# Pair products of a decaying-state attention: one matmul per head on 64 rows of the array, instead of one per pair of heads on 128 rows

## Chip, cores and metric

The kernel runs on one core of one Trainium2 chip. Its metric is the device time of one execution, in microseconds (us); lower is better.

## What is computed

Three layers follow each other. The first is an attention with a decaying state, over 4 batches, 8 heads, 768 steps and 48 channels per head; the other two are dense layers on the 3072 resulting rows of 384 numbers.

```python
for t in range(S):
    kt, vt, rt, wt = (k[:, :, t], v[:, :, t], r[:, :, t], w[:, :, t])
    cur = np.einsum('bhd,bhe->bhde', u[None] * kt, vt)
    y[:, :, t] = np.einsum('bhd,bhde->bhe', rt, state + cur)
    state = wt[:, :, :, None] * state + np.einsum('bhd,bhe->bhde', kt, vt)
...
h = x @ w_in
g = np.where(pos, h, np.where(neg, 0.0, (h + beta) ** 2 / (4.0 * beta)))
x = g @ w_out
...
h = x @ w_in
g = np.where(h > 0.0, h, alpha * (np.exp(np.minimum(h, 0.0)) - 1.0))
out = g @ w_out
```

## The kernel before, in words

**Stages.** The 768 steps are cut into 6 chunks of 128 (`NC = 6`, `CH = 128`). The attention of chunk 0 runs alone ("stage 0" below). Then `layer1_tile(c, True)` computes the first dense layer of chunk c and, woven into it, the attention of chunk c + 1 (stages 1 to 5, c = 0 to 4). Then come the last tile of the first dense layer without attention, and six tiles of the second dense layer.

**Attention of a chunk.** Each batch has 4 pairs of heads. The 16 pairs of a chunk are split into two groups g of `GP = 8`. The tile `att{g}` holds r, w, k with channels on the partitions, a pair of heads at partitions 0 to 47 and 64 to 111 (`PAD = 64`), and steps along the free dimension. The weight that step s has for step t is a product of decays between them; the kernel reaches it in `NL = 7` levels. At level l, with m = 2**l, steps are grouped in blocks of m, and each product of a k in an even block with an r in the odd block behind it is taken. These are the **pair products** (`pair_products`): TensorE multiplies k (stationary, 128 partitions x 128 steps) with odd steps of r (moving). VectorE (`level`) then multiplies odd r by a decay (L777), copies the products that a mask picks from the two PSUM banks into `a_` (two predicated copies, L780), and multiplies even k by a decay (L784); `next_decays` (L791) follows. The next level of the same group needs the updated r and k.

**The block-diagonal copies.** Before, one matmul takes a pair of heads over all 128 partitions. So that the two heads do not mix, its moving operand is `rbd_`, 128 columns per pair: for the upper 64 partitions the first 64 columns hold the 64 odd steps of r and the rest is zero, for the lower ones the other way round. `odd_blocks` fills it with two copies of 64 partitions x 512 elements per level: ScalarE for level 0 of chunk 0 and for levels 1 to 6 (`next_odd_blocks`), GpSimd (`times_one`, L348) for level 0 of later chunks. `wait_rbd` makes TensorE and VectorE wait for them.

**What orders the work.** Each engine's order is written out by hand. `PLAN` gives the slots f (0 to 15) of a dense tile in which levels stand: group 0 in slots 0, 2, 3, 4, 5, 6, 7 ("early", behind `up(c, f)`), group 1 in slots 5 to 11 ("late", behind `down(c, f - 2)`). Rows of the attention itself (`turn_k`, `attend`, `state_step`) stand in slots 9, 10, 13, 14. In slots 5, 6 and 7 both groups have a level. In later chunks both groups share the banks `g_bank`, so `bank_user` also waits for the other group's predicated copies, one half (one bank) at a time. A dense slot is 9 matmuls `up` (three of the moving 512 columns for each of 3 parts of x) and 9 matmuls `down`.

**DMA.** SyncE issues loads and stores (`load_group`, `reload`, `reload_natural`); the change does not touch them.

Of the kernel before, what the change touches and what calls it, by code (L numbers as in the profile page):

```python
# [34 lines left out]
B, H, S, D = 4, 8, 768, 48  # L35
DM, FF = 384, 2048
P = 128
# [10 lines left out]
NL = 7  # L48
# [17 lines left out]
def build(nc, rT, wT, kT, vN, rN, kN, uN, masks_d, ident_d, w1_in, w1_out, w2_in, w2_out, x2_d, out_d):  # L66
    with ExitStack() as ctx:
# [16 lines left out]
        widths = [NR, NR, NR, NR, NV, NA]  # L84
        att = [sb(f"att{g}", [P, sum(widths)]) for g in range(2)]
        r_, w_, k_, rbd_, v_, a_ = ([a[:, sum(widths[:i]):sum(widths[:i + 1])] for a in att]
# [53 lines left out]
        rbd_zeroed = sem("rbd_zeroed")  # L140
        zeroed = sem("zeroed")
        r0_ready = [sem(f"r0_ready{g}") for g in range(2)]
# [13 lines left out]
        rbd_ready = [sem(f"rbd_ready{g}") for g in range(2)]  # L156
# [67 lines left out]
        def odd_blocks(copy, k, g, l):  # L224


            m = 2 ** l
            for a in range(2):
                ps = slice(a * PAD, (a + 1) * PAD)
                if m < HALF:  # L230
                    out = rbd_[g][ps, :].rearrange("p (n a j m) -> p n a j m", a=2, n=GP, m=m)[:, :, a]
                    in_ = r_[g][ps, :].rearrange("p (n j two m) -> p n j two m", n=GP, two=2, m=m)[:, :, :, 1]
                else:
                    out = rbd_[g][ps, :].rearrange("p (n a m) -> p n a m", a=2, m=m)[:, :, a]
                    in_ = r_[g][ps, :].rearrange("p (n two m) -> p n two m", two=2, m=m)[:, :, 1]
                last = copy(out, in_, ps)
            last.then_inc(rbd_ready[g] if l else r0_ready[g], 1)

        def wait_rbd(engine, k, g, l):

            if l == 0:
                engine.wait_ge(r0_ready[g], k + 1)
            else:
                engine.wait_ge(rbd_ready[g], k * (NL - 1) + l)
# [90 lines left out]
        def _(pool):  # L335
# [9 lines left out]
            def times_one(out, in_, ps):  # L345

                ones = consts[ps, 2:3].rearrange("p (x y z) -> p x y z", x=1, y=1)
                return nc.gpsimd.tensor_tensor(out, in_, ones.broadcast_to(list(in_.shape)), ALU.mult)  # L348

# [20 lines left out]
            for g in range(2):  # L370

                nc.gpsimd.memset(rbd_[g], 0.0).then_inc(rbd_zeroed, 1)
            for g in range(2):
                nc.gpsimd.memset(a_[g], 0.0)
# [12 lines left out]
            with pool.Fori(1, NC) as k:  # L387
                for g in range(2):

                    if g == 0:  # L390
                        pool.wait_ge(w1_lo_ready, len(W1_PIECES))
                        pool.wait_ge(vd_ready[1], k)
                    pool.wait_ge(rk_in[g], k * 32 + 32)
                    pool.wait_ge(g_filled[g], k * NFILL)
                    odd_blocks(times_one, k, g, 0)
                pool.wait_ge(r0_ready[1], k + 1)
                for g in range(2):
                    diagonal_product(k, g)
# [6 lines left out]
        def _(pe):  # L405
# [3 lines left out]
            def pair_products(k, g, l):  # L409

                wait_rbd(pe, k, g, l)
                if l == 0:
                    pe.wait_ge(rk_in[g], k * 32 + 32)
                else:
                    pe.wait_ge(k_updated[g], k * NL + l)
                for half in range(2):
                    bank_user(k, g, l, half)
                    bank_ = product_banks(k, g)[half]
                    for i in range(HP):
                        j = half * HP + i  # L420
                        last = mm(bank_[:, i * P:(i + 1) * P], k_[g][:, j * CH:(j + 1) * CH],
                                  rbd_[g][:, j * P:(j + 1) * P])
                    last.then_inc(g_filled[g], 1)

            def bank_user(k, g, l, half):
# [557 lines left out]
```

## Time and profile before

| | |
|---|---|
| median of 3 runs | 1153.86 us |
| lowest and highest run | 1153.84, 1159.4 us |
| span of the profiled execution | 1154.6 us |
| busy, share of span | TensorE matmul 94%, TensorE weight load 79%, VectorE 57%, ScalarE 50%, GpSimd 12% |
| mean granted TensorE clock | 0.980 of full speed |

The profiled execution has no separate time beside its span; 1154.6 us is the time that the steps below are counted against. PE is TensorE's matmuls, PEld its weight loads, DVE VectorE, ACT ScalarE, POOL GpSimd, SPq SyncE's queue. Matmuls overlap one another in the records, so that the distance from one start to the next tells the pace, and the duration of one does not. A float32 matmul of the program shows as two passes in the trace, each with a weight load and a matmul of its own: the 8 matmuls of a level are 16 records.

### The profile page before, as it was taken

Reading aid. Unit: us, or ns where it says so; the run is one execution under the profiler, and the core shown is the slowest. Engines: PE = TensorE matmul, PEld = TensorE weight load, DVE = VectorE, ACT = ScalarE, POOL = GpSimd, SP = SyncE. Lnnn points to the kernel's source line nnn. Section 1 sums busy time; section 2 is a strip of 40 time slices with the busy share of each in tenths; the row PEclk is TensorE's granted clock in tenths of the full one; section 3 lists DMA queues with packets and bytes.
Section 4 is the critical chain, followed back from the end, with each engine's and each line's share of the span. In section 5 each row is a group of like instructions: output and inputs, shape, how many; then the busy total and the mean of one; then the engine's idle time right before and its main releaser. Section 6 shows DMA issues by size and latency. Waiting matters only on the chain.

```text
span 1154.6 us, 15811 instructions
## 1 busy us (share of the span) xinstructions
PE 1086.5 (94%) x5704; PEld 915.1 (79%) x5704; DVE 655.4 (57%) x962; ACT 573.1 (50%) x959; POOL 139.9 (12%) x96
## 2 busy tenths in 40 slices
PE   4687999899989998999989999999999999999998
PEld 3576898689868887788778888888888888888886
DVE  5996855686568656875687544543333333333332
ACT  3444544564456444544454457664545444454543
POOL 5664100310031003100310000000000000000000
PEclk8798999999999999999989999999999999999999
DMA  7233001400140014001400240010101000010000
GB/s 280 85 112 143 1 1 69 150 0 0 68 150 0 0 68 150 0 0 68 150 0 0 109 164 1 4 51 1 54 0 55 0 19 36 0 54 0 27 0 27
DMA packets 23369, 60.58 MB, mean 52 GB/s; under 512 B 2352, under 2 KB 6832, under 8 KB 22960
## 3 DMA queue, kind: packets, MB, share of 16 engines
q1 hardware_dynamic: 23344, 60.27, 14.6%
q8 instruction: 13, 0.21, 0.1%
q14 instruction: 12, 0.10, 0.0%
HBM read 50.82 MB, written 9.44 MB: 52 GB/s over the span
## 4 chain that ended last, share of the span: by engine, by line
PE 85%; DVE 9%; issue 3%; ACT 1%; DMA 1%; SPq 0%; DVEq 0%; ACTq 0%
PE down_bank L407 35%; PE up_bank L407 23%; PE g_bank L407 19%; PE y_bank L407 7%; DVE att L780 4%; DVE att L784 2%; DVE scratch L878 1%; DVE g_lo L848 1%; PE y_bank L447 1%; DMA att<-kT_dram 1%; DVE att L777 1%; PE g_bank L504 0%; DVE att L791 0%; ACT scratch L683 0%; ACT g_hi L607 0%
## 5 line engine op out<-in xcount | busy, mean ns | idle before, releaser
L407 PE MATMUL down_bank<-g_hi,wout_lo 128*128 128x512 f32 x576 | 234.9, 408 | 7.8 <-DVE g_lo L848 7.8
L407 PE MATMUL down_bank<-g_hi,wout_hi 128*128 128x512 f32 x576 | 227.8, 396 | 0.0
L407 PE MATMUL down_bank<-g_lo,wout_hi 128*128 128x512 f32 x576 | 227.6, 395 | 0.0
L607 ACT CAST g_hi<-scratch 128x512 fp32r<-128x512 f32 x192 | 119.1, 621 | 218.4 <-DVE scratch L878 103.0
L407 PE MATMUL g_bank<-att 128*128 128x128 f32 x1232 | 164.1, 288 | 39.4 <-DVE att L784 29.5
L407 PEld LDWEIGHTS g_bank<-att 128*128 128x128 f32 x1232 | 156.4, 201 | 56.0 <-DVE att L780 19.2
L848 DVE TENSOR_TENSOR g_lo<-scratch,g_hi 128x512 fp32r<-128x512 f32 x192 | 141.5, 737 | 87.1 <-ACT g_hi L607 86.0
L407 PE MATMUL up_bank<-x_hi,win_lo 128*128 128x512 f32 x432 | 175.9, 407 | 2.6 <-DVE x_lo L854 2.6
L407 PE MATMUL up_bank<-x_lo,win_hi 128*128 128x512 f32 x432 | 171.4, 397 | 0.0
L407 PE MATMUL up_bank<-x_hi,win_hi 128*128 128x512 f32 x432 | 171.2, 396 | 0.0
L878 DVE SCALAR_TENSOR_TENSOR scratch<-scratch 128x512 f32<-128x512 f32 x96 | 73.5, 765 | 114.1 <-ACT scratch L690 114.1
L607 ACT COPY att<-att 64x512 f32<-64x512 f32 x148 | 92.6, 626 | 91.9 <-DVE att L777 87.7
L407 PEld LDWEIGHTS down_bank<-g_hi,wout_lo 128*128 128x128 f32 x576 | 109.1, 189 | 30.9 <-DVE g_lo L848 9.0
L407 PEld LDWEIGHTS down_bank<-g_hi,wout_hi 128*128 128x128 f32 x576 | 108.7, 189 | 25.6
L780 DVE COPY_PREDICATED att<-masks,g_bank 128x512 f32<-128x512 int32 x154 | 127.5, 894 | 0.3
L407 PEld LDWEIGHTS down_bank<-g_lo,wout_hi 128*128 128x128 f32 x576 | 109.1, 189 | 21.8
L407 PEld LDWEIGHTS up_bank<-x_hi,win_lo 128*128 128x128 f32 x432 | 82.2, 190 | 19.8 <-DVE x_lo L854 2.9
L407 PEld LDWEIGHTS up_bank<-x_hi,win_hi 128*128 128x128 f32 x432 | 82.0, 190 | 19.3
L407 PEld LDWEIGHTS up_bank<-x_lo,win_hi 128*128 128x128 f32 x432 | 82.2, 190 | 17.1
L777 DVE TENSOR_TENSOR att<-att 128x512 f32<-128x512 f32 x84 | 69.1, 823 | 45.0 <-PE g_bank L407 42.7
L902 DVE SCALAR_TENSOR_TENSOR scratch<-scratch,up_bank 128x512 f32<-128x512 f32 x48 | 33.0, 688 | 100.7 <-ACT scratch L717 100.7
L683 ACT ACTIVATE scratch<-up_bank,consts 128x512 f32<-128x512 f32 x96 | 66.1, 688 | 44.1 <-PE up_bank L407 43.4
(75 smaller groups left out, 1257.8 us busy)
## 6 DMA issues: line engine op xcount, KB each, us to landing
att<-rT_dram SPq DMA_DIRECT2D x12, 512.0 KB, 3.5
att<-kT_dram SPq DMA_DIRECT2D x12, 512.0 KB, 4.3
att<-wT_dram SPq DMA_DIRECT2D x12, 512.0 KB, 6.1
ynat<-rN_dram SPq DMA_DIRECT2D x12, 384.0 KB, 5.2
k_steps<-kN_dram SPq DMA_DIRECT2D x12, 384.0 KB, 6.1
att<-vN_dram SPq DMA_DIRECT2D x12, 384.0 KB, 6.5
x_dram<-scratch SPq DMA_DIRECT2D x18, 256.0 KB, 3.8
ynat<-x_dram SPq DMA_DIRECT2D x6, 768.0 KB, 4.3
```

The costliest lines, as they stand in the source:

```text
L407: return nc.tensor.matmul(out, lhsT, rhs, start=start, stop=stop, **kw)
L447: last = nc.tensor.transpose(banks(k, b)[0][:, i * P:(i + 1) * P], k_[g][:, j * CH:(j + 1) * CH], ident[:, :])
L607: return nc.scalar.copy(out, in_)
L683: nc.scalar.activation(act_buf[f % 2], up_bank[f % 2][:, :], ACT.Relu, bias=consts[:, 0:1], scale=0.5).then_inc(p_ready, 1)
L777: nc.vector.tensor_tensor(r[:, :, 1, :], r[:, :, 1, :], w[:, :, 0, 0:1].broadcast_to(shape), ALU.mult).then_inc(r_updated[g], 1)
L780: nc.vector.copy_predicated(a[:, half, :].rearrange("p (n two m) -> p n two m", two=2, m=m)[:, :, 1, :], masks[:, l:l + 1, :].broadcast_to ...
L784: nc.vector.tensor_tensor(kk[:, :, 0, :], kk[:, :, 0, :], w[:, :, 1, 0:1].broadcast_to(shape), ALU.mult).then_inc(k_updated[g], 1)
L848: nc.vector.tensor_tensor(g_lo[:, f % 2, :], act_buf[f % 2], g_hi[:, f % 2, :].bitcast(F32), ALU.subtract).then_inc(glo_ready, 1)
L878: nc.vector.scalar_tensor_tensor(out=act_buf[f % 2], in0=act_buf[f % 2], scalar=1.0, in1=qbuf, op0=ALU.min, op1=ALU.add).then_inc(g_ready, 1)
L902: nc.vector.scalar_tensor_tensor(out=act_buf[f % 2], in0=act_buf[f % 2], scalar=-1.0, in1=up_banks2[f % 4][:, :], op0=ALU.add, op1=ALU.max ...
```

## The change

It does away with `rbd_` and everything that fills it or waits for it (`odd_blocks`, `wait_rbd`, `next_odd_blocks`, `times_one`, three kinds of semaphores, two memsets). `pair_products` now issues, for each of the 8 pairs and each head a of it, a matmul on 64 partitions only, with 64 moving columns read from `r_` in place (`odd_steps`). The products of the first heads go to the first bank and those of the second heads to the second bank, one right behind the other, so index n of `a_` becomes `a * GP + j`. The waits for the banks are taken once per level, for both halves together (`bank_users`).

```diff
-        widths = [NR, NR, NR, NR, NV, NA]
-        att = [sb(f"att{g}", [P, sum(widths)]) for g in range(2)]
-        r_, w_, k_, rbd_, v_, a_ = ([a[:, sum(widths[:i]):sum(widths[:i + 1])] for a in att]
+        widths = [NR, NR, NR, NV, NA]
+        att = [sb(f"att{g}", [P, max(sum(widths), KT * FF)]) for g in range(2)]
+        r_, w_, k_, v_, a_ = ([a[:, sum(widths[:i]):sum(widths[:i + 1])] for a in att]
...
+        def odd_steps(g, l, a, j):
+            return both_levels(r_[g][a * PAD:(a + 1) * PAD, j * CH:(j + 1) * CH], 2 ** l)[:, :, 1, :]
...
-            for g in range(2):
-                nc.gpsimd.memset(rbd_[g], 0.0).then_inc(rbd_zeroed, 1)
...
                     if g == 0:
                         pool.wait_ge(w1_lo_ready, len(W1_PIECES))
-                        pool.wait_ge(vd_ready[1], k)
-                    pool.wait_ge(rk_in[g], k * 32 + 32)
-                    pool.wait_ge(g_filled[g], k * NFILL)
-                    odd_blocks(times_one, k, g, 0)
-                pool.wait_ge(r0_ready[1], k + 1)
-                for g in range(2):
+                    pool.wait_ge(vd_ready[g], k)
                     diagonal_product(k, g)
...
-                wait_rbd(pe, k, g, l)
                 if l == 0:
                     pe.wait_ge(rk_in[g], k * 32 + 32)
                 else:
+                    pe.wait_ge(r_updated[g], k * NL + l)
                     pe.wait_ge(k_updated[g], k * NL + l)
-                for half in range(2):
-                    bank_user(k, g, l, half)
-                    bank_ = product_banks(k, g)[half]
-                    for i in range(HP):
-                        j = half * HP + i
-                        last = mm(bank_[:, i * P:(i + 1) * P], k_[g][:, j * CH:(j + 1) * CH],
-                                  rbd_[g][:, j * P:(j + 1) * P])
-                    last.then_inc(g_filled[g], 1)
+                bank_users(k, g, l)
+                for j in range(GP):
+                    for a in range(2):
+                        last = mm(product_banks(k, g)[a][:, j * PAD:(j + 1) * PAD],
+                                  k_[g][a * PAD:(a + 1) * PAD, j * CH:(j + 1) * CH], odd_steps(g, l, a, j))
+                        if j == GP - 1:
+                            last.then_inc(g_filled[g], 1)
...
                 if l > 0:
-                    pe.wait_ge(masked[g], k * NFILL + 2 * (l - 1) + half + 1)
+                    pe.wait_ge(masked[g], k * NFILL + 2 * l)
...
                 if later(k) and other:
-                    pe.wait_ge(masked[1 - g], k * NFILL + 2 * other[-1] + half + 1)
+                    pe.wait_ge(masked[1 - g], k * NFILL + 2 * other[-1] + 2)
...
-                        n, e = 2 * j + a, slice(j * E2 + a * D, j * E2 + (a + 1) * D)
+                        n, e = a * GP + j, slice(j * E2 + a * D, j * E2 + (a + 1) * D)
...
-                    if level[1] is not None and level[1] >= 1:
-                        next_odd_blocks(k, 1, level[1])
-                if part == "late":
-                    if level[0] is not None and level[0] + 1 < NL:
-                        next_odd_blocks(k, 0, level[0] + 1)
```

What follows is how the instructions stand on TensorE around a level of group 1 in a slot that has a level of each group, behind the nine `down` matmuls and ahead of the nine `up` matmuls. Before:

```order
L407 MATMUL down_bank<-g_hi,wout_hi 128x512
L433 REGISTER_ALU
L407 MATMUL g_bank<-att 128x128 x4
L433 REGISTER_ALU
L407 MATMUL g_bank<-att 128x128 x4
L530 REGISTER_ALU
L407 MATMUL up_bank<-x_hi,win_lo 128x512
```

After:

```order
L372 MATMUL down_bank<-g_hi,wout_hi 128x512
L397 REGISTER_ALU
L372 MATMUL g_bank<-att 128x64 x16
L494 REGISTER_ALU
L372 MATMUL up_bank<-x_hi,win_lo 128x512
```

The place in the program is the same; the 8 matmuls of 128 columns became 16 of 64, and the second wait, between the two banks, is gone.

On ScalarE, the same slot of stages 1 to 5. Before, two pairs of copies into `rbd_` (`att<-att`) stand around the work of the dense tile:

```order
L607 COPY att<-att 64x8x64 x2
L607 CAST g_hi<-scratch 128x512
L607 COPY att<-att 64x8x64 x2
L683 ACTIVATE scratch<-up_bank,consts 128x512
L687 ACTIVATE scratch<-up_bank,consts 128x512
L690 ACTIVATE scratch<-scratch 128x512
```

After:

```order
L571 CAST g_hi<-scratch 128x512
L634 ACTIVATE scratch<-up_bank,consts 128x512
L638 ACTIVATE scratch<-up_bank,consts 128x512
L641 ACTIVATE scratch<-scratch 128x512
```

Only the copies went; the order of the rest is unchanged.

## Rows read from the trace of the kernel before

**Rows 1.** The page: span, engines, and the chain that ended last, by engine.
```profile
span 1154.6 us, 15811 instructions
PE 1086.5 (94%) x5704; PEld 915.1 (79%) x5704; DVE 655.4 (57%) x962; ACT 573.1 (50%) x959; POOL 139.9 (12%) x96
PE 85%; DVE 9%; issue 3%; ACT 1%; DMA 1%; SPq 0%; DVEq 0%; ACTq 0%
```

**Rows 2.** Busy time by stage; each engine with its instructions, then the granted clock.
```profile
0.00:94.00 94.00, 58.47 (x376) 54.67 (x377) 73.30 (x93) 38.65 (x68) 58.85 (x50) 0.85 0.50 172
327.20:444.00 116.80, 111.63 (x670) 96.08 (x669) 79.94 (x124) 58.23 (x99) 17.21 (x10) 1.00 0.15 54
680.00:747.00 67.00, 67.00 (x290) 54.03 (x289) 32.60 (x42) 47.77 (x76) 0.00 (x0) 1.00 0.12 43
```

**Rows 3.** PE in order of time, a level between two `up`s: start, us, operation.
```profile
329.05 0.39 PE L407 MATMUL up_bank<-x_hi,win_hi 128*128 128x512 f32 x1
329.28 1.95 PE L407 MATMUL g_bank<-att 128*128 128x128 f32 x16
330.98 0.48 PE L407 MATMUL up_bank<-x_hi,win_lo 128*128 128x512 f32 x1
331.30 0.39 PE L407 MATMUL up_bank<-x_lo,win_hi 128*128 128x512 f32 x1
331.53 0.39 PE L407 MATMUL up_bank<-x_hi,win_hi 128*128 128x512 f32 x1
```

**Rows 4.** PE in order of time, two heads' part of an `attend`.
```profile
314.30 0.43 PE L407 MATMUL y_bank<-state,att 128*128 128x96 f32 x2
314.57 0.57 PE L407 MATMUL y_bank<-att 128*128 128x48 f32 x4
314.97 0.43 PE L407 MATMUL y_bank<-state,att 128*128 128x96 f32 x2
```

**Rows 5.** The tile g_bank: count, duration ns min/median/max.
```profile
L407 PEld LDWEIGHTS g_bank<-att x1232: 186/192/338, 8.2 to 650.6; 128*128 128x128 f32 x176
L407 PE MATMUL g_bank<-att x1232: 270/275/578, 8.2 to 650.7; 128*128 128x128 f32 x176
```

**Rows 6.** Stage 3 in order of time: where PE and DVE wait at its head.
```profile
331.29 0.69 DVE L878 SCALAR_TENSOR_TENSOR scratch<-scratch 128x512 f32<-128x512 f32 x1 [4.79 <-ACT scratch L690]
331.90 0.69 DVE L777 TENSOR_TENSOR att<-att 128x512 f32<-128x512 f32 x1
336.90 2.05 PE L407 MATMUL g_bank<-att 128*128 128x128 f32 x16 [1.49 <-DVE att L784]
341.25 0.50 PE L407 MATMUL down_bank<-g_hi,wout_lo 128*128 128x512 f32 x1 [2.30 <-DVE g_lo L848]
346.80 2.05 PE L407 MATMUL g_bank<-att 128*128 128x128 f32 x16 [1.11 <-DVE att L784]
```

**Rows 7.** The same stage, slot 5: weight loads of group 1's level, in two halves.
```profile
366.83 0.97 PEld L407 LDWEIGHTS g_bank<-att 128*128 128x128 f32 x8 [0.53 <-issue]
367.99 0.97 PEld L407 LDWEIGHTS g_bank<-att 128*128 128x128 f32 x8 [0.19 <-issue]
```

**Rows 8.** Groups by line: copies into rbd_ and its memsets; busy us, mean ns.
```profile
L607 ACT COPY att<-att 64x512 f32<-64x512 f32 x148 | 92.6, 626 | 91.9 <-DVE att L777 87.7 <-DMA att<-kT_dram 3.2
L348 POOL TENSOR_TENSOR att<-att,consts 64x512 f32<-64x512 f32 x20 | 23.6, 1179 | 294.7 <-DMA att<-kT_dram 294.1
L372 POOL MEMSET att<- 128x1024 f32 x2 | 1.8, 952 | 0.0
```

**Rows 9.** Stage 0 in order of time.
```profile
8.25 3.75 PE L407 MATMUL g_bank<-att 128*128 128x128 f32 x16 [8.25 <-ACT att L607]
11.38 1.32 ACT L607 COPY att<-att 64x512 f32<-64x512 f32 x2 [3.23 <-DMA att<-kT_dram]
12.75 3.67 PE L407 MATMUL down_bank<-att 128*128 128x128 f32 x16 [0.75 <-ACT att L607]
...
43.57 1.73 DVE L777 TENSOR_TENSOR att<-att 128x512 f32<-128x512 f32 x1
47.20 2.02 PE L407 MATMUL g_bank<-att 128*128 128x128 f32 x16
47.44 1.74 DVE L777 TENSOR_TENSOR att<-att 128x512 f32<-128x512 f32 x1
```

More of the change, by code:

```diff
@@ L139, in build @@
         tile_stored = sem("tile_stored")
-        rbd_zeroed = sem("rbd_zeroed")
         zeroed = sem("zeroed")
-        r0_ready = [sem(f"r0_ready{g}") for g in range(2)]
         rk_multiplied = [sem(f"rk_multiplied{g}") for g in range(2)]
@@ L155, in build @@
         decay_ready = [sem(f"decay_ready{g}") for g in range(2)]
-        rbd_ready = [sem(f"rbd_ready{g}") for g in range(2)]
         kt_filled = sem("kt_filled")
@@ L222, in both_levels @@
             return ap.rearrange("p (n two m) -> p n two m", two=2, m=m)
[L224 to L244, printed above, removed]
+        def odd_steps(g, l, a, j):
+            return both_levels(r_[g][a * PAD:(a + 1) * PAD, j * CH:(j + 1) * CH], 2 ** l)[:, :, 1, :]
         @block.sync
@@ L343, in rows @@
                 return buf[:, 2 * g:2 * g + 2, :]
-            def times_one(out, in_, ps):
-                ones = consts[ps, 2:3].rearrange("p (x y z) -> p x y z", x=1, y=1)
-                return nc.gpsimd.tensor_tensor(out, in_, ones.broadcast_to(list(in_.shape)), ALU.mult)
             def diagonal_product(k, g):
@@ L414, in pair_products, with bank_users @@
                 else:
+                    pe.wait_ge(r_updated[g], k * NL + l)
                     pe.wait_ge(k_updated[g], k * NL + l)
-                for half in range(2):
-                    bank_user(k, g, l, half)
-                    bank_ = product_banks(k, g)[half]
-                    for i in range(HP):
-                        j = half * HP + i
-                        last = mm(bank_[:, i * P:(i + 1) * P], k_[g][:, j * CH:(j + 1) * CH],
-                                  rbd_[g][:, j * P:(j + 1) * P])
-                    last.then_inc(g_filled[g], 1)
-            def bank_user(k, g, l, half):
+                bank_users(k, g, l)
[5 more added lines that the diff above has]
+                            last.then_inc(g_filled[g], 1)
+            def bank_users(k, g, l):
                 other = [i for i, f in enumerate(PLAN[1 - g]) if (f, 1 - g) < (PLAN[g][l], g)]
                 if l > 0:
-                    pe.wait_ge(masked[g], k * NFILL + 2 * (l - 1) + half + 1)
-                elif g == 0 and later(k) and half == 0:
+                    pe.wait_ge(masked[g], k * NFILL + 2 * l)
+                elif g == 0 and later(k):
                     pe.wait_ge(xlo_ready, k * B)
                 if later(k) and other:
-                    pe.wait_ge(masked[1 - g], k * NFILL + 2 * other[-1] + half + 1)
+                    pe.wait_ge(masked[1 - g], k * NFILL + 2 * other[-1] + 2)
             def turn_k(k, b):
@@ L638, in w2_hi_of @@
                         copy(hi, raw).then_inc(w2_hi_ready, 1)
-            def copy_odd(out, in_, ps):
-                return copy(out, in_)
-            def next_odd_blocks(k, g, l):
-                act.wait_ge(g_filled[g], k * NFILL + 2 * l)
-                act.wait_ge(r_updated[g], k * NL + l)
-                odd_blocks(copy_odd, k, g, l)
             def attention(k, f, part, plan=PLAN):
@@ L725, in layer2_tile @@
                     x2_hi_of(x_next, m)
-            for g in range(2):
-                act.wait_ge(rbd_zeroed, g + 1)
-                act.wait_ge(rk_in[g], 32)
-                odd_blocks(copy_odd, 0, g, 0)
             act.wait_ge(zeroed, 1)
@@ L772, in level @@
                     dve.wait_ge(decay_ready[g], k * NL + l)
-                wait_rbd(dve, k, g, l)
                 w, r, kk = (both_levels(x[g], m) for x in (w_, r_, k_))
```

## The prediction

> **What bounds the kernel now.** I read the page first. TensorE is busy for 94% of the span, and 85% of the chain that ended last lies on it [rows 1]. The reader is to see two things: no other engine is near, and what matters is how long TensorE is occupied, not how much work ScalarE has.
>
> The stage table comes next [rows 2]. Stage 0, attention alone, has TensorE busy for 58.5 of 94 us and VectorE for 73.3, so VectorE is the fuller engine there. Stage 3, which stands for stages 1 to 5, lasts 116.8 us with TensorE busy for 111.6 at full clock, VectorE for 79.9 and ScalarE for 58.2. The tile without attention lasts 67.0 us. So weaving the attention in costs 49.8 us per stage, nearly all TensorE's own time: 5.2 us is idle. The second dense layer takes the rest of the span and holds none of the changed instructions.
>
> Then the pace of a level. It starts at 329.28 and the next matmul at 330.98: 1.70 us for 16 passes, 0.106 us each [rows 3]. A stage has 14 levels, thus 23.8 us of them, and stages 1 to 5 have 70.
>
> **What limits a pass.** This is the question of the whole change, because it doubles the passes of a level (16 matmuls, 32 passes) and halves their moving columns. In `attend`, 6 passes with 96 and 48 moving columns take from 314.30 to 314.97, 0.67 us, or 0.112 us each [rows 4]. Passes with 128, 96 or 48 columns thus all come about 0.11 us apart. The moving columns do not set the pace; something that each pass has once does. A pass has one weight load of 128 columns, 192 ns long and overlapped with its neighbours [rows 5]. The change halves what costs nothing here and doubles what sets the pace.
>
> The Trainium skill says (TensorE: Matmul & The Clock Gate, "LDWEIGHTS") that a weight load costs by its columns and that the rows do not count; no row here has a load of 64 rows, so that half of the rule is not shown by this trace.
>
> **The sum, part by part.**
>
> 1. *Passes.* 32 x 0.106 = 3.40 us for a level instead of 1.70. The nearest rows are full-height passes; passes on half of the rows, for which loads or streams on the other half might run at once, appear nowhere in the trace. Lower bound: the two heads overlap fully and each pass costs its 64 columns only, half of a 128-column pass, 16 x 0.053 = 0.85 us a level, 0.85 less than now. Upper bound: nothing overlaps, and passes keep their distance: 3.40. I take 3.40, since the passes of `attend` [rows 4], the nearest in columns, did not get closer. 70 levels x 1.70 = **+119.0**.
> 2. *Entering and leaving half-height mode.* Where the kind of matmul changes, 0.32 us pass between two starts instead of 0.23 [rows 3], thus 0.09. The change of height comes at the same places. Bounds: nothing, and one full matmul length of 0.275 [rows 5] on each side, 0.55 a level or 38 us. I take 0.09 per level, the row that shows a change of kind: 70 x 0.09 = **+6.3**. The Trainium skill says (TensorEngine Tiling, "Key Properties") that changing the tiling mode drains TensorE; by it this term would be nearer to its upper bound. No trace here shows it.
> 3. *What TensorE's waits absorb.* At the head of a stage it waits 1.49 and 1.11 us for VectorE's k update and 2.30 us for g_lo, 4.9 together [rows 6]. The first level ends at about 331.2 (its last pass 0.2 after 330.98), but VectorE takes it up at 331.90, behind L878 [rows 6]: 0.7 us of the first 1.7 is free. The second level's 1.7 eats into the 2.30, as VectorE works through its queue meanwhile. I count 2.6 us a stage at the head. In slots 5 and 6 group 1's level waits in two halves, 0.53 and 0.19 [rows 7]; with TensorE slower, VectorE is ahead and these 0.4 us twice go as well. (If TensorE did not get slower, the single wait for both banks would instead hold the first half back by up to 0.7 us, twice a stage, 7 us in all.) 5 x (2.6 + 0.8) = **-17**.
> 4. *ScalarE's copies.* 148 copies of 626 ns, 92.6 us, go [rows 8]. TensorE waits for VectorE at the places of step 3, and ScalarE has half of each stage free [rows 2], so I cost this at **0**. The cover is TensorE's own work; without it, a pair of copies between g_hi and the activations would be worth 1.3 us on that chain. GpSimd's 20 multiplications of level 0, 23.6 us, sit in the tail of a stage, before their level is due: **0**.
> 5. *Stage 0.* The second group starts at 12.75, behind ScalarE's two copies that began at 11.38 when k had landed [rows 9]. Without them it starts 1.4 us sooner. The first group starts up to 2.6 us sooner (8.25; of it 1.8 from the two memsets [rows 8, 9]), hidden behind the second. From then on VectorE works on one group while TensorE makes the products of the other. Around 43 to 47 us VectorE comes around every 3.87 us (43.57 to 47.44) [rows 9]; 3.4 us of passes and two hand-overs of some 0.15 just fill it, and the granted clock is 0.85 on the mean there [rows 2]: at its lower level, 1.2 GHz, a level already takes some 3.7 us (8.25, 12.75) and would stick out. Bounds -3 and +20; I take +5 for the later levels, less 1.4: **+4**.
>
> Sum: 119.0 + 6.3 - 17 + 0 + 4 = +112. Against the 1154.6 us of the profiled execution, which stands 0.7 above the median of the runs (1153.86), that gives **1267 us**.
>
> **Rivals.**
>
> *A. Loads of the two heads overlap, streams too, but a load still takes 0.106 (about the same time).* The two heads of a pair use different rows and different banks and are issued alternately. If the two loads run side by side, a pair of passes costs what one costs now and a level stays at 1.70. Then remain the changes of mode (6 to 21 us by step 2, the upper figure for 0.3 a level), up to 7 us for the single wait, and -1.4 to -3 in stage 0: 1154 to 1180 us, 1166 in the middle. For it: rows and banks do not conflict. Against it: no record shows two loads at once. The Trainium skill states this rule (TensorEngine Tiling, "Key Properties": different tiles can execute weight loads and matmuls in parallel); whether it holds for two loads, no trace here tells.
>
> *B. In between.* The loads overlap in part, or issuing so many short instructions limits: 2.0 to 3.2 us a level. With 0.3 to 1.5 us more on 70 levels, 21 to 105, and the absorption of step 3: 1175 to 1250 us.
>
> *C. The other side: the pace is set by streams, not loads, and two heads stream at once.* A level takes 0.85 us. It decides if half-height loads go below 53 ns a pass. Four of the 14 levels of a stage (slots 0, 2, 5, 6) are ones behind which VectorE is awaited and would give nothing back, so 10 x 0.85 x 5 = 42 us, and 1.4 in stage 0: 1111 us. Against it stand the passes of 48 columns at 0.112 [rows 4]: a stream half as long did not help there.
>
> *D. The change does not do what it says:* the two heads do not overlap at all. That is my forecast, in fact, not a rival; it would be worse only if each switch between the halves drained the array. Then a pass would cost its whole 0.275 and the time would pass 1500 us. I give it 2 in 100.
>
> **How the numbers follow.** The forecast (no overlap, 3.4 us a level): 0.52. B 0.15, A 0.22, C 0.09, D 0.02. About 0.5%, 5.8 us, is what a measurement of this kernel tells from no change. Of A I put 0.08 within it and 0.02 below. Faster 0.11, same 0.08, slower 0.81. The forecast's own range is 1240 to 1290: step 2 at its bounds (-6, +32), step 5 (-7, +16), step 3 half or one and a half times (8 each way), not all at once. The range for 8 in 10 starts at 1157, leaving out C and the low part of A, and ends at 1290.
>
> **What would show it.** Right: in the profile after, 32 passes of 64 columns from first start to the next operation's start in 3.3 to 3.6 us, weight loads one behind the other at 0.106; stages of about 138 us instead of 117; the waits at the head of a stage below 3 us; VectorE no busier; ScalarE at about 480 us. Wrong: two weight loads starting within 20 ns of each other and 1.7 us a level (A), or less (C); or stage lengths near 117 us. If levels take 3.4 us and the stages grow by under 18 us, step 3 is what failed. If stage 0 ends before 94 us, step 5.

## The result, and the profile after

| | before | after |
|---|---|---|
| median of 4 runs | 1153.85 us | 1224.33 us |
| lowest and highest | 1153.59, 1159.4 | 1216.23, 1226.39 |
| span of the profiled execution | 1154.6 us | 1221.6 us (its time: 1223.38) |
| ratio after to before | | 1.0559, 95% interval 1.0487 to 1.063 |

The change makes the kernel 5.6% slower by the ratio of the runs; the medians differ by 70 us, the two spans by 67. The medians below are of all runs of a kernel, while the ratios leave out the few executions that fell into a second, slower state (one of the four of a_heads_apart, one of the twelve of b_filled0 and two of the kernel before). The page of the kernel after, to be read against [rows 1], with its line on the clock and that on the queue which loads TensorE's instructions (packets, MB, share):

```profile
span 1221.6 us, 18116 instructions
PE 1151.9 (94%) x7048; PEld 956.3 (78%) x7048; DVE 647.2 (53%) x962; ACT 482.6 (40%) x811; POOL 111.8 (9%) x74
PEclk9999899989998999899989999999999999999999
q8 instruction: 56, 0.92, 0.3%
PE 88%; DVE 6%; issue 4%; ACT 1%; DMA 1%; SPq 0%; DVEq 0%; ACTq 0%
```

TensorE is again busy for 94% and has 65 us more to do; its passes went from 5704 to 7048, by the 1344 that the change adds. ScalarE lost the 90 us of its copies, and that shortened nothing. "issue" rose from 3% to 4% of the chain, and the instruction queue moved 0.92 MB; before it moved this:

```profile
q8 instruction: 13, 0.21, 0.1%
```

Three stretches make up the 67 us. The first dense tile starts at 101.3 us instead of 88.0 (stage 0: +13.3). The five stages with attention, up to the start of the tile without it, last 645.3 us instead of 593.5 (+51.8), and the rest 475.0 instead of 473.1. The table of stretches of the kernel after for stage 0 and for stages 1 to 5, then the second of them before (columns as in [rows 2]; the granted clock of 1.00 in the first line is no reading, see below):

```profile
0.00:99.50 99.50, 76.87 (x572) 74.89 (x572) 71.32 (x89) 20.46 (x37) 54.68 (x44) 1.00 0.42 144
101.30:746.60 645.30, 604.31 (x4460) 503.35 (x4461) 395.16 (x620) 215.58 (x372) 57.13 (x30) 0.95 0.15 54
```
```profile
88.00:681.50 593.50, 565.23 (x3340) 486.12 (x3341) 403.53 (x620) 289.72 (x492) 83.33 (x49) 0.98 0.16 58
```

Then a level, in order of time: its first passes in a view of 0.04 us, and the whole of it with its neighbours (to be read against [rows 3]):

```profile
391.60 0.40 PE L372 MATMUL up_bank<-x_hi,win_hi 128*128 128x512 f32 x1
391.93 0.19 PEld L372 LDWEIGHTS g_bank<-att 64*128 64x128 f32 x2 [0.36 <-issue]
391.93 0.33 PE L372 MATMUL g_bank<-att 64*128 64x64 f32 x2
...
391.93 2.00 PE L372 MATMUL g_bank<-att 64*128 64x64 f32 x32
393.86 0.50 PE L372 MATMUL down_bank<-g_hi,wout_lo 128*128 128x512 f32 x1
394.20 0.39 PE L372 MATMUL down_bank<-g_lo,wout_hi 128*128 128x512 f32 x1
```

Two weight loads and two matmuls start within the same 0.01 us: one of each head. The level goes in such pairs: 32 passes take 1.93 us to the next operation, not 3.40. (In some levels the two starts of a pair lie 0.04 us apart instead; the level is as long.) So the loads of the two heads do run side by side; this was rival A's rule, not the forecast's. A load on 64 rows is as long as one on 128 was [rows 5], 0.19 us. The starts of single passes in this stretch are 0.112 us apart from pair to pair, as they are from pass to pass before. The level is nevertheless 0.23 us longer than the 1.70 of before. The step into it takes 0.10 more (391.60 to 391.93, 0.33 instead of 0.23), and the two operations behind it start 0.34 apart instead of 0.32. Together that is 0.35 us a level; b_last_half below shows that the change of height is worth about as much.

TensorE's longest waits after:

```profile
PE g_bank L372 <- DVE att L726: 16.3, 10, 2.2
PE g_bank L372 <- DVE att L730: 14.9, 7, 4.2
PE up_bank L372 <- issue: 9.4, 4, 2.4
PE down_bank L372 <- DVE att L730: 7.5, 4, 2.6
PE g_bank L372 <- issue: 6.2, 4, 3.8
```

Each row gives what TensorE waited for, the us in total, how often, and the longest. The first row is new: ten waits for the predicated copies (L726, L780 before), twice in each of the five stages. The rows with "issue" are new as well, 15.6 us in eight places at or just behind the head of four stages. They don't simply add to the time: within the stages TensorE's waits for VectorE at the heads shrank meanwhile, from 29.5 us (the two lines below, and 2.6 for x_lo) to 11.4.

```profile
PE g_bank L407 <- DVE att L784: 19.1, 10, 5.2
PE down_bank L407 <- DVE g_lo L848: 7.8, 4, 2.3
```

One of each of the new waits, in order of time:

```profile
363.87 0.61 PE L372 MATMUL up_bank<-x_hi,win_lo 128*128 128x512 f32 x1 [2.30 <-issue]
370.33 2.31 PE L372 MATMUL g_bank<-att 64*128 64x64 f32 x22 [1.75 <-issue]
...
406.37 2.42 DVE L726 COPY_PREDICATED att<-masks,g_bank 128x512 f32<-128x512 int32 x2
408.91 1.89 PEld L372 LDWEIGHTS g_bank<-att 64*128 64x128 f32 x32 [2.60 <-issue]
408.94 2.00 PE L372 MATMUL g_bank<-att 64*128 64x64 f32 x32 [2.19 <-DVE att L726]
```

At 408.94 the level of group 1 starts only when both predicated copies of group 0 are done (406.37 + 2.42 = 408.79), where before it began with one bank after the first copy [rows 7]. The copies are 1.3 us long each and overlap a little; the first is done at 407.65.

Stage 0, the chain of the kernel after, and the same two steps before:

```profile
65.69 3.41 PE g_bank L372 x32
69.11 3.41 PE down_bank L372 x32
72.52 1.04 PE up_bank L411 x4
73.56 3.28 PE down_bank L372 x16
76.84 1.79 PE g_bank L372 x8
```
```profile
72.10 1.72 PE down_bank L407 x16
73.82 0.93 PE g_bank L407 x8
```

The rows of attention, which the change leaves as they are, take twice as long: 3.28 instead of 1.72, and together 25.8 us (72.52 to 98.33) instead of 13.5 (71.48 to 85.02). TensorE's clock is at its lower level, 1.2 GHz. The clock line prints a 9 there, and the table a 1.00, only because this trace's first clock record stands at 104.7 us; until then the operations go at half the pace, a level of 32 passes in 3.41 us instead of 1.93. Before, the first record is one of the upper level at 16.2 us, and 40 of the 88 us were at the lower one. In the stages too the clock is lower than before: by the clock records, 64.8 us of the 645.3 are at the lower level (3.4 of them ahead of the first record), against 20.4 of the 593.5. TensorE was busy in 62.3 and 15.7 us of them.

### The profile page after: what moved, and what is told of

The parts are those of the page before. It is cut to its first block, busy times and chain, and to the rows that moved or that the text cites. A ratio compares the mean times of both kernels' runs of the same rounds, so it can differ in the third digit from the quotient of the medians.

```text
span 1221.6 us, 18116 instructions
## 1 busy us (share of the span) xinstructions
PE 1151.9 (94%) x7048; PEld 956.3 (78%) x7048; DVE 647.2 (53%) x962; ACT 482.6 (40%) x811; POOL 111.8 (9%) x74
## 4 chain that ended last, share of the span: by engine, by line
PE 88%; DVE 6%; issue 4%; ACT 1%; DMA 1%; SPq 0%; DVEq 0%; ACTq 0%
PE down_bank L372 36%; PE up_bank L372 23%; PE g_bank L372 20%; PE y_bank L372 7%; DVE att L726 4%; DVE att L730 1%; PE y_bank L411 1%; DVE att L737 1%; DMA att<-kT_dram 1%; DVE att L723 0%; PE g_bank L468 0%; PE up_bank L411 0%; DVE g_lo L794 0%; SPq L233 0%; ACT scratch L634 0%
## 5 line engine op out<-in xcount | busy, mean ns | idle before, releaser
L372 PE MATMUL down_bank<-g_hi,wout_lo 128*128 128x512 f32 x576 | 239.8, 416 | 2.2 <-DVE g_lo L794 2.2
L372 PE MATMUL down_bank<-g_hi,wout_hi 128*128 128x512 f32 x576 | 232.1, 403 | 0.0
L372 PE MATMUL down_bank<-g_lo,wout_hi 128*128 128x512 f32 x576 | 231.1, 401 | 0.0
L372 PEld LDWEIGHTS g_bank<-att 64*128 64x128 f32 x2464 | 162.4, 207 | 71.6 <-issue 61.8
L372 PE MATMUL g_bank<-att 64*128 64x64 f32 x2464 | 173.5, 294 | 43.2 <-DVE att L726 16.3
L372 PE MATMUL up_bank<-x_hi,win_lo 128*128 128x512 f32 x432 | 180.6, 418 | 11.8 <-issue 9.4
L794 DVE TENSOR_TENSOR g_lo<-scratch,g_hi 128x512 fp32r<-128x512 f32 x192 | 135.1, 704 | 89.3 <-ACT g_hi L571 88.2
L372 PEld LDWEIGHTS down_bank<-g_hi,wout_hi 128*128 128x128 f32 x576 | 110.8, 192 | 27.3
L824 DVE SCALAR_TENSOR_TENSOR scratch<-scratch 128x512 f32<-128x512 f32 x96 | 69.0, 719 | 118.8 <-ACT scratch L641 118.6
L726 DVE COPY_PREDICATED att<-masks,g_bank 128x512 f32<-128x512 int32 x154 | 126.8, 891 | 0.3
L723 DVE TENSOR_TENSOR att<-att 128x512 f32<-128x512 f32 x84 | 75.0, 893 | 83.2 <-PE g_bank L372 81.6
L848 DVE SCALAR_TENSOR_TENSOR scratch<-scratch,g_bank 128x512 f32<-128x512 f32 x48 | 33.1, 689 | 80.4 <-ACT scratch L668 80.4
```

The source lines that it names most:

```text
L372: return nc.tensor.matmul(out, lhsT, rhs, start=start, stop=stop, **kw)
L723: nc.vector.tensor_tensor(r[:, :, 1, :], r[:, :, 1, :], w[:, :, 0, 0:1].broadcast_to(shape), ALU.mult).then_inc(r_updated[g], 1)
L726: nc.vector.copy_predicated(a[:, half, :].rearrange("p (n two m) -> p n two m", two=2, m=m)[:, :, 1, :], masks[:, l:l + 1, :].broadcast_to ...
L794: nc.vector.tensor_tensor(g_lo[:, f % 2, :], act_buf[f % 2], g_hi[:, f % 2, :].bitcast(F32), ALU.subtract).then_inc(glo_ready, 1)
L824: nc.vector.scalar_tensor_tensor(out=act_buf[f % 2], in0=act_buf[f % 2], scalar=1.0, in1=qbuf, op0=ALU.min, op1=ALU.add).then_inc(g_ready, 1)
L848: nc.vector.scalar_tensor_tensor(out=act_buf[f % 2], in0=act_buf[f % 2], scalar=-1.0, in1=up_banks2[f % 4][:, :], op0=ALU.add, op1=ALU.max ...
```

## The experiments

Each stands beside its own runs of the kernel before, whose medians lay between 1153.3 and 1156.0 us. "Stages" below is the time from the start of the first dense tile to that of the tile without attention: 593.5 before, 645.3 after.

### b_two_columns_halves: as many passes, at full height

```diff
-                        last = mm(bank_[:, i * P:(i + 1) * P], k_[g][:, j * CH:(j + 1) * CH],
-                                  rbd_[g][:, j * P:(j + 1) * P])
+                        for a in range(2):
+                            last = mm(bank_[:, i * P + a * PAD:i * P + (a + 1) * PAD], k_[g][:, j * CH:(j + 1) * CH],
+                                      rbd_[g][:, j * P + a * PAD:j * P + (a + 1) * PAD])
```

> The kernel before, with each pair product cut into two matmuls of 64 columns that keep all 128 partitions: as many instructions and passes as the change has, but full height. Theory H (height): the passes do not overlap and keep their 0.112 us, so a level goes from 1.8 to 3.6 us, +125 us on 70 levels less some 17 that waits absorb; TensorE's program is as long as the change's, so its code is loaded anew in every stage (instruction queue about 56 packets instead of 13) and TensorE stands 2.3 us at four stage heads; the granted clock however is at its upper level in stage 0 from 20 to 60 us on, since the passes are full height. 1265 to 1290 us. Theory N (number): only the number of instructions counts, then stage 0 stays at the lower clock until 100 us as in the change, and a level of 32 passes takes the change's 1.9 us: about 1225 us.

Measured: 1326.55 us, ratio 1.1472 (1.1399 to 1.1545). In order of time, a level in a stage and two in stage 0:

```profile
464.80 3.68 PE L407 MATMUL g_bank<-att 128*128 128x64 f32 x32
468.29 0.48 PE L407 MATMUL down_bank<-g_hi,wout_lo 128*128 128x512 f32 x1
...
62.84 7.03 PE L407 MATMUL g_bank<-att 128*128 128x64 f32 x32
69.67 7.04 PE L407 MATMUL down_bank<-att 128*128 128x64 f32 x32
```

A level takes 3.49 us (464.80 to 468.29): full-height passes with half the columns do not come closer than 0.11 us. So a pass's moving columns don't set its pace, as the prediction had it, and it is the two row halves that make the overlap of the changed kernel. The instruction queue moves 56 packets as in the changed kernel: that goes with the number of instructions, not the height. My expectation on the clock was wrong: stage 0 runs at 6.83 us a level (62.84 to 69.67), twice 3.41, with TensorE busy all the time, and the first clock record comes at 135.7 us. The low clock is thus not a matter of half height alone. Stage 0 is 44.6 us longer than before (132.6 us); this is what puts it 37 us over the upper end of what I expected, since the stages grew by 130 us.

### b_single_wait: the change's waits in the kernel before

```diff
+                bank_users(k, g, l)
                 for half in range(2):
-                    bank_user(k, g, l, half)
...
-                    pe.wait_ge(masked[1 - g], k * NFILL + 2 * other[-1] + half + 1)
+                    pe.wait_ge(masked[1 - g], k * NFILL + 2 * other[-1] + 2)
```

> The kernel before with the change's single wait for both banks. If the single wait matters (in slots 5 and 6 TensorE stands until the second predicated copy is done): 0.7 to 1.1 us at two levels of 5 stages, +6 to +11 us, 1160 to 1165. If it is hidden: 1152 to 1156.

Measured: 1179.67 us, ratio 1.022 (1.0157 to 1.0283): +24 us by the medians, more than twice what I expected. Its waits:

```profile
PE g_bank L407 <- DVE att L784: 29.7, 14, 4.8
PE g_bank L407 <- DVE att L780: 18.7, 10, 2.5
```

Ten waits, 18.7 us, for the second predicated copy; in the changed kernel the same ten cost 16.3 (above). Its stages take 615.7 us, +22.2. With the change of height (b_last_half) this is the largest cost that the change brought, and it has nothing to do with how fast the matmuls are. In the change as it stands it goes with the overlap: the two heads write to different banks at the same time, so each level begins in both banks at once. Copying by pairs of heads across both banks, so that the first half of both came free sooner, is not possible without TensorE writing a bank that VectorE is reading; that was not run.

### a_unrolled: TensorE's loop written out

```diff
-            with pe.Fori(0, NC - 1) as c:
+            for c in range(NC - 1):
                 layer1_tile(c, True)
```

> The changed kernel with TensorE's loop over the five tiles with attention written out, so that its code is read straight on and never jumps back. Theory L (code loading): the 15.6 us of issue waits at four stage heads go, with most of the clock dips behind them: 1195 to 1208 us, no issue wait over 1 us. Rival: the waits come from something else at the stage heads (DMA traffic, VectorE): 1218 to 1227 us.

Measured: 1208.39 us (1203.17 to 1214.56), ratio to before 1.0457 (1.0379 to 1.0535), against 1.0559 of the changed kernel. Of the issue waits, this is left:

```profile
PE g_bank L372 <- issue: 1.6, 2, 1.2
```

15.6 us became 1.6, and the stages take 633.3 us instead of 645.3. It is just above the upper end of what I expected. Most of the clock dips behind the heads did not go with the waits: 54.6 us of the stages are at the lower level, against 64.8. Nor are the 12 us simply the waits that went. TensorE waits 10 us more for VectorE at the heads instead (21.6 against 11.4), so that only 4.0 of the 12 are less idle time; the other 8.0 are less busy time (596.3 against 604.3), where the clock comes in.

### b_unrolled: the same in the kernel before

> The kernel before with TensorE's loop over the five tiles with attention written out. Its loop was read once and stayed (no instruction packets between 195 and 688 us), so writing it out can only add code reading. Theory L: reading straight on is hidden, 1152 to 1158 us, and the gain of a_unrolled is due to the change's longer code. Rival: jumping back costs in the kernel before as well: 1135 to 1148 us.

Measured: 1155.45 us, ratio 0.9996 (0.9967 to 1.0025), over 10 runs. Writing the loop out does nothing by itself: it brings small issue waits, 5.8 us in the stages, in the place of waits for VectorE (11.5 us for L784 instead of 19.1). Before, the loop's code was read once (no packet on the instruction queue between 195 and 688 us); in the changed kernel some ten packets come in every stage. So the change seems to have pushed the loop past the length that stays loaded, and each jump back then waited for code; a_half_count below, whose code is as short as before, has no such wait.

### a_filled0: full-height work in stage 0

```diff
+FILL = 2
...
+                        if f < NL and part != "middle":
+                            for _ in range(FILL):
+                                mm(up_bank[0][:, 0:DM], ident[:, :], u_nat[:, :])
```

The first level of both groups moved with it, ahead of the wait for the constants that the fillers read.

> The changed kernel with 4 filler matmuls (full height, 384 columns) behind the levels of each of the slots 0 to 6 of stage 0, where TensorE waits for VectorE anyway; their result is not used. Theory C (clock): half-height passes do not count for the clock; with the fillers the upper level is granted before 60 us and the first dense tile starts near 90 instead of 101 us: 1210 to 1216 us. Rival: the clock is low there for another reason and the fillers only delay: first tile at 101 us or later, 1224 us or more.

Measured: 1209.19 us (1202.16 to 1218.93), ratio 1.0447 (1.0374 to 1.052). The chain in the profiled execution (of 1217.1 us):

```profile
69.93 3.61 PE down_bank L373 x32
73.54 2.67 PE up_bank L373 x4
76.21 1.93 PE g_bank L373 x32
78.14 1.49 PE up_bank L373 x4
```

The clock rose at 17.9 us, was low again from 31.5 to 38.3 and from 45.2 to 75.9, and stayed up for the rest of stage 0. The rows of attention then took 13.3 us (83.05 to 96.4) instead of 25.8 (72.52 to 98.33). In this execution the fillers themselves (2.67 and 1.49 us for four in the lines above, 2.86 in the slots ahead of them) ate that up: the first tile started at 99.4. So the clock costs the changed kernel 12.4 us in these rows, but this run alone doesn't show that it can be had back. Its issue waits are also down, to 3.8 us from 15.6, though its loop is not written out; and yet its stages take 643.0 us, 2.3 less than those of the changed kernel. The waits for VectorE grew in their place here too.

### a_unrolled_filled0: both

> The changed kernel with TensorE's loop written out and the fillers in stage 0, both. Code loading and the clock of stage 0 are separate costs: a_unrolled alone took 1208, and a_filled0 brought the first dense tile from 101.3 to 99.4 us, so 1204 to 1208 us if its other gain (1209 against 1224) was a luckier code loading; if the gains add up in full: 1193 us.

Measured: 1199.4 us (1191.16 to 1203.31), ratio 1.0386 (1.0335 to 1.0437). In the profiled execution (span 1189.4) only 30 us of stage 0 were at the lower clock and the first tile started at 90.4 instead of 101.3. Between my two expectations: how much the fillers give back varies from one execution to the next, and with it how long the clock stays low (55 us of stage 0 in a_filled0, 30 here). This is the best version of the changed kernel, and still 3.9% slower than the kernel before.

### a_heads_apart: same matmuls, other order

```diff
-                for j in range(GP):
-                    for a in range(2):
+                for a in range(2):
+                    for j in range(GP):
```

> The changed kernel with the same 16 matmuls of a level in another order: first the eight of the upper 64 rows, then the eight of the lower, so that neighbours share rows. Theory O (overlap needs alternating heads): loads no longer run in pairs, a level takes 32 x 0.112 = 3.6 us instead of 1.93, +1.65 on 70 levels, less 20 to 30 us of waits that go under: 1300 to 1320 us. Rival: the engine overlaps any two half-height passes, or pulls loads ahead across the order: level stays below 2.3 us, 1220 to 1245 us.

Measured: 1389.93 us, ratio 1.1961 (1.1853 to 1.207), 70 above what I expected. A level with its neighbours, then single passes ahead of the change of rows and at it, each in a view of a few hundredths of a us:

```profile
397.18 0.40 PE L372 MATMUL down_bank<-g_hi,wout_hi 128*128 128x512 f32 x1
397.51 3.39 PE L372 MATMUL g_bank<-att 64*128 64x64 f32 x32
400.82 0.50 PE L372 MATMUL up_bank<-x_hi,win_lo 128*128 128x512 f32 x1
...
398.11 0.50 PE L372 MATMUL g_bank<-att 64*128 64x64 f32 x3
398.89 0.49 PE L372 MATMUL g_bank<-att 64*128 64x64 f32 x5
```

A level takes 3.32 us: the overlap needs neighbours on different rows. On the same rows the passes follow at 0.112 us, as full-height ones do: three within 0.50 us, the last of them 0.27 long. Only where the rows change, in the middle of the level, do a few starts come closer (five within 0.49 us): there the first passes on the lower rows run beside the last ones on the upper rows. That is why the level is 0.26 us short of 32 x 0.112. So the engine does reach across the order, but not further than these few passes. The rest of the excess is the clock. Its stages spend 242 us at the lower level, against 65 in the changed kernel, and the dense tile's own matmuls slow down with it.

### a_half_count: half as many half-height matmuls

```diff
-                    for a in range(2):
-                        last = mm(product_banks(k, g)[a][:, j * PAD:(j + 1) * PAD],
-                                  k_[g][a * PAD:(a + 1) * PAD, j * CH:(j + 1) * CH], odd_steps(g, l, a, j))
+                    a, n = j % 2, j // 2
+                    last = mm(product_banks(k, g)[a][:, n * CH:(n + 1) * CH],
+                              k_[g][a * PAD:(a + 1) * PAD, j * CH:(j + 1) * CH],
+                              r_[g][a * PAD:(a + 1) * PAD, j * CH:(j + 1) * CH])
...
```

> The changed kernel with 8 half-height matmuls of 128 columns per level, alternating between upper and lower rows, instead of 16 of 64. It computes the products of one head of each pair only and leaves the others out. As many instructions as before the change. Theory L: TensorE's code stays resident (13 to 20 packets on the instruction queue), no issue waits at stage heads. Theory S (short passes keep the clock down, not half height): with 128 columns the upper level is granted before 60 us. A level takes 8 pairs x 0.112 and 0.4 for the changes of height, about 1.3 us. Time by both: 1130 to 1160 us. If half height keeps the clock down: stage 0 low throughout, 10 to 12 us more; if the code is loaded anew in spite of its length: issue waits of 2 us at four heads.

It leaves out the products of one head of each pair. Measured: 1143.05 us, ratio 0.9861 (0.9791 to 0.9931). Its instruction queue and a level:

```profile
q8 instruction: 13, 0.21, 0.1%
...
263.48 1.16 PE L372 MATMUL g_bank<-att 64*128 64x128 f32 x16 [1.21 <-DVE att L727]
264.57 0.50 PE L372 MATMUL down_bank<-g_hi,wout_lo 128*128 128x512 f32 x1
```

13 packets and no issue wait: the code loading is a matter of the number of instructions. The level takes 1.09 us, eight pairs and the change of height. The clock stayed at the lower level throughout stage 0 (first record at 101.8 us), with 128 columns too. So neither short passes nor half height alone explain it: without fillers, stage 0 stayed low both with full-height passes of 64 columns and with half-height passes of 64 or 128, and the clock rose at 13 to 16 us in the kernels whose levels are full-height passes of 128, wholly or, in b_last_half, but for one matmul in eight. Even with half of the products gone, the gain over the kernel before is only 13 us.

### b_last_half: one matmul in eight at half height

```diff
+                        rows = slice(0, PAD if j == GP - 1 else P)
-                        last = mm(bank_[:, i * P:(i + 1) * P], k_[g][:, j * CH:(j + 1) * CH],
-                                  rbd_[g][:, j * P:(j + 1) * P])
+                        last = mm(bank_[:, i * P:(i + 1) * P], k_[g][rows, j * CH:(j + 1) * CH],
+                                  rbd_[g][rows, j * P:(j + 1) * P])
```

> The kernel before, with the last of the eight matmuls of each level on the upper 64 rows only (still 128 columns): the products of the second head of one pair in eight are left out. It adds a change of height and back to each level and nothing else: same instructions, same passes, separate waits per bank. If a change of height costs what the changed kernel's trace suggests (0.1 us going in and 0.2 to 0.25 coming out): +0.3 on 70 levels, 1172 to 1180 us. Rival: the longer gaps in the changed kernel are due to its wait or its short passes: 1152 to 1158 us. On the clock: if any half-height passes keep it down in stage 0, the upper level comes only after 85 us; if only a level made of them does, as in before, near 16 us.

Measured: 1185.15 us (1175.96 to 1187.5), ratio 1.0221 (1.014 to 1.0301), 5 us above what I expected. The levels begin as before; this is a whole one and what follows it:

```profile
375.46 2.14 PE L407 MATMUL g_bank<-att 128*128 128x128 f32 x16
377.53 0.50 PE L407 MATMUL down_bank<-g_hi,wout_lo 128*128 128x512 f32 x1
377.86 0.39 PE L407 MATMUL down_bank<-g_lo,wout_hi 128*128 128x512 f32 x1
```

A level takes 2.07 us instead of 1.70 to 1.78, with the same number of passes. Its stages take 619.9 us, +26.4, and stage 0 +4.5. The change of height is thus a cost by itself, of 0.3 to 0.4 us there and back. The clock rose at 14.2 us, with two half-height passes among the sixteen of each level.

### b_pool_later and b_filled0: two tries at beating both

The kernel before waits at the head of a stage while GpSimd and VectorE run side by side [rows 6]. Held back by one more wait (and the diagonal's sums moved from slots 4 and 5 to 6 and 7):

```diff
+                pool.wait_ge(k_updated[0], k * NL + 2)
                 for g in range(2):
                     diagonal_product(k, g)
...
```

> The kernel before, with GpSimd's four multiplications for the diagonal held back until VectorE is through level 1 of group 0 (slot 2), and their sums moved from slots 4 and 5 to 6 and 7. In the trace of before they run beside VectorE at the head of each stage, where its operations take 1.9 to 2.3 us instead of 0.7 and TensorE waits 4.9 us. If those waits are due to that and slots 3 and 4 have room: 2 to 4 us less per stage, 1135 to 1147 us. Rival: VectorE is stretched in slots 3 and 4 just as much and TensorE waits there: 1150 to 1160 us.

Measured: 1158.68 us over 12 runs, ratio 1.0021 (0.999 to 1.0052). In order of time:

```profile
352.50 2.36 DVE L849 TENSOR_TENSOR g_lo<-scratch,g_hi 128x512 fp32r<-128x512 f32 x1
354.78 2.33 DVE L778 TENSOR_TENSOR att<-att 128x512 f32<-128x512 f32 x1
```

VectorE's operations are stretched to the same 2.3 us beside GpSimd's, which now begin 15 us into the stage instead of 5; the rival had it. The fillers in the kernel before:

> The kernel before with the fillers of a_filled0 in stage 0. If the lower clock in stage 0 (40 us of 88) costs time: the first dense tile starts 2 to 4 us sooner, 1149 to 1153 us. Rival: VectorE sets stage 0 in the kernel before, its last part is at full clock already, and the fillers bring nothing or delay: 1153 to 1160 us.

Measured: 1156.67 us over 12 runs, ratio 1.001 (0.9983 to 1.0036). Its profiled execution has 18.7 us at the lower clock in stage 0 instead of 40, and starts the first tile at 86.3 instead of 88.0; the gain doesn't show in the time, which the rival had. Neither beats the kernel before, which remains the fastest complete one.

## Why the prediction was right and wrong

The sign was right and 1224 lies in the range, in the stretch from 1175 to 1250 that I gave to rival B. But the time came about in another way than in any of my cases, and my likeliest mechanism was wrong. That 1224 lies in the range is luck: costs that I had small or not at all came in the place of the one large term that did not come.

**Step 1, passes (+119): failed.** "What limits a pass" was right as far as it is shown: full-height passes come 0.11 us apart, whatever their moving columns (b_two_columns_halves, 3.49 us a level). That it is the weight load that sets this pace is likely but not shown, since every load in these runs has 128 columns. The wrong step was to take the nearest full-height row as evidence that passes on different rows would not overlap either. They do: pairs at 0.112 us. The term is 0 instead of +119. The rule of the Trainium skill (TensorEngine Tiling, "Key Properties"), that tiles load weights and multiply in parallel, stood beside rival A; the trace after agrees with it for two loads at once. I had 0.22 on it.

**Step 2, change of height (+6.3): mis-sized.** The trace after has 0.10 going in, 0.23 more for the level and 0.02 between the next two: 0.35 a level, 24 us for 70. b_last_half, which adds nothing else, comes to +26 in the stages. The upper bound that I had (0.55) held it; the row that I took, a change of number format, was not near enough. The same page of the Trainium skill says that changing the tiling mode drains TensorE; the trace after has a cost at both changes, but less than a matmul's length of 0.275 at each, and nothing that shows a drain as such.

**Step 3, what waits absorb (-17): wrong sign.** Since the levels did not get slower, there was little to absorb, and the single wait that I had put into brackets at 7 us costs 22 in the stages (24 by the medians) when made alone. I had counted 0.7 us for each of ten levels; the ten waits themselves come to 18.7 us. A predicated copy is 1.3 us long there, as in the changed kernel (above), and the second is done 1.1 us after the first (408.79, 407.65 there), so 0.7 was too little. The stages of b_single_wait also have 27.3 us at the lower clock instead of 20.4. In slots 5 and 6 the two groups' levels take turns on VectorE and TensorE, so that a late start is probably passed on to the next level; that part is argued and not measured by itself.

**Step 4, ScalarE's and GpSimd's copies (0): right.** 90 and 28 us of busy time went, and no stage got shorter.

**Step 5, stage 0 (+4): mis-sized, and for another reason.** It grew by 13.3. The clock, of which I had only thought within the levels, stayed low to the end and doubled rows that the change does not touch: 25.8 us instead of 13.5 before, 12.3 us; a_filled0, where the clock was up, has 13.3 for the same rows. The levels ahead of them, for which the +4 stood, end 1.0 us later than before (72.52 against 71.48).

**Not foreseen: the length of the code.** 112 more matmuls in the loop body made TensorE wait 15.6 us for instructions; written out, the kernel is 16 us faster by the medians, 12 in the stages. How much of the 12 is the waits themselves stays open: only 4.0 of it is less idle time, and in a_filled0 most of these waits are gone without the stages being much shorter.

**Not foreseen: the clock in the stages.** They have 44 us more at the lower level than before, with TensorE busy nearly throughout. At the upper level such work takes half the time, so that this is worth up to (62.3 - 15.7) / 2 = 23 us, an estimate from the clock records and busy times above.

So the terms are: stage 0 +13.3; stages: change of height 24, single wait 22, code 12, together 58 where 52 are seen; the rest +2. The three are from runs that make each alone, and that they come within 6 us of 52 does not close the account, because the clock is in it too. TensorE's time in the stages can be split another way: of the 52, 39 are busy time (604.3 instead of 565.2) and 13 idle (41.0 instead of 28.3). In the idle time the two new waits, 16.3 and 15.6, stand against 18.1 less waiting for VectorE. In the busy time the change of height leaves some 15 us, for which the lower clock is the one cause at hand. A part of the clock's cost is inside the three terms (27.3 us at the lower level in b_single_wait, 23.9 in b_last_half, 54.6 in a_unrolled); no run separates the rest.

What stays open: why the clock stays down in stage 0, and why it falls more often in the stages of the changed kernel.

## What to carry to other kernels

Splitting a matmul into two that use half of the rows each gained nothing here, where passes keep 0.112 us from one to the next whatever their moving columns: the two halves overlap only as long as they alternate, and then they just reach the pace that one full-height matmul had. Against that stand a change of height at every entry and exit (0.35 us here), two banks that must be free at the same time, and twice the instructions. Before adding instructions to a long hand-written loop, look at the instruction queue: if it is silent during the loop, as it was before, the loop's code stays loaded; where packets come in every stage, look for waits at each jump back. And read how long TensorE was at its lower clock in each stage of both kernels before adding up other causes.

## What was not expected of the hardware

- Two half-height passes on different rows start within 0.01 to 0.04 us of each other, loads included, and pairs follow at 0.112 us; on the same rows single passes follow at 0.112 us.
- TensorE can be busy nearly all the time and stay at 1.2 GHz: in b_two_columns_halves for the first 132 us, with matmuls in 122 of them. (The 1.00 for the clock in this line is again that of a stretch ahead of the first record; the pace of 6.83 us a level there, against 3.49 later, shows the level.)

```profile
0.00:132.60 132.60, 122.08 (x573) 121.70 (x573) 63.54 (x92) 37.01 (x65) 53.39 (x48) 1.00 0.31 108
```

- What stands in front of a stretch can decide its clock: the same rows of attention took 25.8 us in the changed kernel and 13.3 in a_filled0, which differs in the fillers ahead of them.
